# Recurrent attention and a mixture of experts in one kernel: waits moved off TensorE, another order of the opening, and split scores for the fourth unit

## The reference

```python
m_new = np.maximum(f_gate[:, :, t] + m, i_gate[:, :, t])
f_stab = np.exp(f_gate[:, :, t] + m - m_new)
i_stab = np.exp(i_gate[:, :, t] - m_new)
C = f_stab[:, :, None, None] * C + i_stab[:, :, None, None] * np.einsum('bhd,bhe->bhde', vt, kt)
n = f_stab[:, :, None] * n + i_stab[:, :, None] * kt
h_tilde = np.einsum('bhde,bhe->bhd', C, qt)
denom = np.maximum(np.abs(nq), 1.0)          # nq = n . q
y[:, :, t] = sigmoid(o_gate[:, :, t]) * h_tilde / denom
...
h = np.maximum(x @ w1[e], 0.0)               # for each of 4 experts
out += p[:, e:e + 1] * (h @ w2[e])           # p: domain_probs, normalised
```

## Time and profile before

| | |
|---|---|
| median of 3 runs | 418.74 us (417.88 to 418.81) |
| the profiled execution's own time | 418.08 us |
| its span, first to last instruction | 416.4 us |
| outside the span | 1.7 us |
| PE busy | 411.6 us, 99% |
| PE weight loads | 398.3 us, 96% |
| DVE, ACT, POOL busy | 43%, 38%, 37% |

### The profile page before, as it was taken

The page is one execution under the profiler, slowest core; times in us unless marked ns, Lnnn a source line. Parts: engine busy times, 40 slices in busy tenths (PEclk is TensorE's granted clock), DMA queues, the critical chain, the costliest instruction groups (busy, mean ns, idle before and its releaser), DMA issues.

```text
span 416.4 us, 7050 instructions
## 1 busy us (share of the span) xinstructions
PE 411.6 (99%) x2710; PEld 398.3 (96%) x2710; DVE 180.6 (43%) x372; ACT 158.5 (38%) x329; POOL 152.3 (37%) x189
## 2 busy tenths in 40 slices
PE   8999999999999999999999999999999999999997
PEld 8899999999999999999999999999999999999996
DVE  5875796646555556446223232323113132311313
ACT  4575477745355653514112431144211333211111
POOL 4865735595174925304011660065100453000000
PEclk9999999999999999999999999999999999999999
DMA  7999939678513845300000231024200000000101
GB/s 269 272 283 394 369 100 354 226 256 290 189 37 131 303 132 193 122 2 0 2 0 2 85 129 67 0 71 139 71 0 2 0 0 2 34 0 2 63 0 65
DMA packets 16899, 48.45 MB, mean 116 GB/s; under 512 B 1921, under 2 KB 8594, under 8 KB 15714
## 3 DMA queue, kind: packets, MB, share of 16 engines
q1 hardware_dynamic: 16290, 46.60, 31.9%
q10 hardware_dynamic: 576, 1.40, 1.0%
HBM read 45.94 MB, written 2.05 MB: 115 GB/s over the span
## 4 chain that ended last, share of the span: by engine, by line
PE 98%; DVE 1%; issue 0%; DVEq 0%
PE hid_ps L1076 42%; PE acc_ps L1095 37%; PE out_ps L1032 5%; PE score_ps L1095 3%; PE acc_ps L1076 2%; PE out_ps L1039 2%; PE score_ps L976 2%; PE add_ps L1011 1%; PE hid_ps L925 1%; PE score_ps L971 1%; PE acc_ps L1032 0%; PE out_ps L1051 0%; PE out_ps L1052 0%; PE out_ps L1053 0%; PE score_ps L989 0%
## 5 line engine op out<-in xcount | busy, mean ns | idle before, releaser
L810 DVE SCALAR_TENSOR_TENSOR h_lo<-hid_ps,h_hi 128x384 fp32r<-128x384 f32 (+2 forms) x120 | 68.0, 567 | 219.7 <-ACT h_hi L587 219.6
L587 ACT ACTIVATE h_hi<-hid_ps 128x384 fp32r<-128x384 f32 (+2 forms) x120 | 59.6, 497 | 231.9 <-PE hid_ps L1076 231.8
L1095 PE MATMUL acc_ps<-w_hi,h_hi 128*128 128x320 f32 x352 | 110.2, 313 | 0.0
L1095 PE MATMUL acc_ps<-w_hi,h_lo 128*128 128x320 f32 x352 | 108.8, 309 | 0.0
L1095 PE MATMUL acc_ps<-w_lo,h_hi 128*128 128x320 f32 x352 | 108.4, 308 | 0.0
L1076 PE MATMUL hid_ps<-xt_hi,w_hi 128*128 128x384 f32 (+2 forms) x360 | 104.1, 343 | 0.1
L1076 PE MATMUL hid_ps<-xt_hi,w_lo 128*128 128x384 f32 (+2 forms) x360 | 103.7, 342 | 0.0
L441 POOL TENSOR_TENSOR w_lo<-w_raw,w_hi 128x384 fp32r<-128x384 f32 x56 | 58.9, 1054 | 114.5 <-ACT w_hi L573 114.5
L1076 PEld LDWEIGHTS hid_ps<-xt_hi,w_lo 128*128 128x128 f32 x360 | 65.4, 189 | 4.3
L1095 PEld LDWEIGHTS acc_ps<-w_hi,h_hi 128*128 128x128 f32 x352 | 66.3, 188 | 1.3
L1095 PEld LDWEIGHTS acc_ps<-w_lo,h_hi 128*128 128x128 f32 x352 | 66.3, 188 | 1.3
(11 more groups left out here) (172 smaller groups left out, 371.9 us busy)
## 6 DMA issues: line engine op xcount, KB each, us to landing
w_raw<-in_w_b SPq DMA_DIRECT2D x27, 704.0 KB, 4.3
raw<-in_qk_s SPq DMA_DIRECT2D x8, 1024.0 KB
g_all<-g_dram SPq DMA_DIRECT2D x10, 512.0 KB, 6.1
kv<-in_kv_n SPq DMA_DIRECT2D x12, 352.0 KB, 5.9
q_pack<-in_q_p SPq DMA_DIRECT2D x10, 192.0 KB, 6.1
out_y<-y_acc SPq DMA_DIRECT2D x12, 160.0 KB, 1.8
carry<-g_dram SPq DMA_DIRECT2D x30, 60.0 KB
y_acc<-in_o_n SPq DMA_DIRECT2D x1, 1280.0 KB, 12.3
```

The source lines that it names most:

```text
L587: nc.scalar.activation(h_hi[:, M % RING, 0:cols], hid_bank(M)[:, 0:cols], ACT.Relu).then_inc(hid_hi, 1)
L810: nc.vector.scalar_tensor_tensor(h_lo[:, M % RING, 0:cols], hid_bank(M)[:, 0:cols], 0.0, h_hi[:, M % RING, 0:cols].bitcast(fp32), ALU.max, ...
L1095: last = nc.tensor.matmul(acc_ps[t][:, 0:DM], x, w, start=(f == 0 and i == 0), stop=(f == NF - 1 and i == 2))
```

## The change

It has four parts.

1. **Waits.** `up` no longer waits for `hid_lo` (that the hidden bank's last reader is done); an assertion in the program says that a `down` before it has waited for as much. It waits for `xt_hi_done` and `xt_done` only where a group brings new tiles. `scores` waits once per unit for its input. `additions` and `outputs` of units from 2 on wait for the keys' weights, the probabilities and the scaled queries alone; what else they waited for is now waited for by DVE ahead of the second `probs` of the unit, and by POOL ahead of `weigh_keys` and `scale_q`. Counted over the whole program, PE has 668 waits before and 432 now, and the waits beyond one at an instruction, which stand in its sequencer as instructions of their own, are 185 before and 73 now.
2. **The opening.** PE moves the chunk ends and starts (`move_ends`, `move_starts`) before the first scores, runs `keep_clock(6)` between the first scores and `outputs(0)`, and turns the first keys into another bank (`hid_ps[0]` in place of `acc_ps[2]`), copied by ACT (`first_keys`) in place of DVE. DVE does `unit_maxima` before the four first `probs`, then `unit_steps` (from POOL) and `gate_scan(1)`, then both `gate_x`. POOL does `unit_sums` between the two `weigh_keys`. ACT rounds weight blocks 2 and 3 before the first transposes, and opens output gates 2 and 3 between the two first `relu`.
3. **Unit 3.** NS is 3 in place of 4: unit 3 takes the layout `qk_s`, with CAST in slots 3 and 4 and SUB in 4 and 5. Its input is loaded on ACT's queue in the opening (`load_scores(act, 3)`, 1 MB), not on SP's after `load_g(3)` (0.4 MB in two transfers). SP issues weight pair 3 before it waits for the stored gates.
4. **Rows.** `state` and `split_qk` have 120 partitions in place of 128, and the state's product in `outputs` runs over the 120 or 80 rows that are in use. Four memsets go (two of POOL's, for unit 3's old layout; one of DVE's, for the rows left out; POOL's memset of `state` covers 120 partitions).

```diff
-NS = 4
+NS = 3
+CAST = {3: (3, 4), 4: (11, 12), ...
+SUB = {3: (4, 5), 4: (13, 14), ...
-OPEN_IN = {3: (2,), 13: (4,), 14: (6,), 17: (8,), 18: (10,)}
+OPEN_IN = {13: (4,), 14: (6,), 17: (8,), 18: (10,)}
...
             sp.dma_start(g_dram[1, NU:NU + 1, :], gate_tiles[1]["gg"][0:1, 1, :]).then_inc(gate_tiles[1]["stored"], 16)
-            load_q(3)
+            load_pair(sp, 3)
             sp.wait_ge(gate_tiles[1]["stored"], 3 * 16)
             load_g(2)
+            load_carry(2)
+            load_q(3)
             sp.wait_ge(out_done, 1)
             sp.wait_ge(add_done, 1)
             load_kv(sp, 2)
-            load_carry(2)
-            load_pair(sp, 3)
             load_g(3)
-            reload_scores(3)
...
+            def first_keys():
+                gt = gate_tiles[0]
+                act.wait_ge(gt["key_ps"], 1)
+                nc.scalar.activation(key_w[:, 0:U0], hid_ps[0][:, U0:2 * U0], ACT.Copy).then_inc(gt["key_tok"], 1)
...
             split_high(1, None)
+            first_keys()
             act.dma_start(y_acc[:, 2:4, :], o_n[:, 2:4, :]).then_inc(o_in[1], 16)
             act.dma_start(dp[:, :, :], dom_p).then_inc(dp_in, 16)
+            load_scores(act, 3)
+            split_high(2, None)
+            split_high(3, None)
             xt_high(0)
             xt_high(1)
-            split_high(2, None)
-            split_high(3, None)
             relu(0)
+            gate_open(2)
             relu(1)
...
                 wait_if(dve, out_done, k - 1)
+                if k >= B and half == 1:
+                    dve.wait_ge(fresh_ready, k)
+                    dve.wait_ge(xt_done, k)
+                if k == B and half == 1:
+                    dve.wait_ge(decay_step, 3)
...
             local_maxima()
             unit_starts()
+            unit_maxima()
...
             probs(0, 0)
             probs(0, 1)
-            unit_maxima()
             probs(1, 0)
             probs(1, 1)
-            copy_keys(0, 0, U0, acc_ps[2])
+            unit_steps()
+            gate_scan(1)
             gate_x(0)
-            gate_scan(1)
             gate_x(1)
...
                 if first_of_load(M):
                     pe.wait_ge(w_hi_done, NF * load + f + 1)
-                if f == 0:
+                if f == 0 and new_tiles(M // NF):
                     pe.wait_ge(xt_hi_done, first + tiles)
-                wait_if(pe, hid_lo, hid_free(M))
...
             exponents_first(0, 1)
+            move_ends()
             exponents_first(1, 0)
             exponents_first(1, 1)
-            move_ends()
+            move_starts()
             first_scores(0)
-            move_starts()
             first_scores(1)
+            pe.wait_ge(m_begun, 1)
+            keep_clock(6)
             outputs(0)
             pe.wait_ge(g0["exp"], 1)
             pe.wait_ge(g0["w_tok"], 1)
-            turn(g0, "key", acc_ps[2], U0, U0, "key_ps")
+            turn(g0, "key", hid_ps[0], U0, U0, "key_ps")
             outputs(1)
             transpose_x(0)
             additions(0)
+            pe.wait_ge(g0["key_tok"], 1)
             keep_clock(2)
```

More of the change, by code:

```diff
@@ L71, in begun_in, with down_before, new_tiles @@
     return None if M == EARLY - 2 or ahead >= SLOTS else ahead
+def down_before(M):
+    slots = [at for at in range(SLOTS) if begun_in(at) == M]
+    return slots[0] if slots else 0
+def new_tiles(at):
+    return at == 0 or GROUPS[at][1] + GROUPS[at][2] > max(g[1] + g[2] for g in GROUPS[:at])
 def hid_free(M):
@@ L231, in build @@
         d_exp, d_masked, p_ready = sem("d_exp"), sem("d_masked"), sem("p_ready")
-        mask_turn, ones_set, apart_set = sem("mask_turn"), sem("ones_set"), [sem(f"apart_set{i}") for i in range(2)]
+        mask_turn, ones_set, apart_set = sem("mask_turn"), sem("ones_set"), sem("apart_set")
         kv_ones, unit_step, first_in = sem("kv_ones"), sem("unit_step"), [sem(f"first_in{i}") for i in range(B)]
@@ L265, in scores_in @@
         def scores_in(k):
-            return 16 * (k // 2 + 1)
+            return 16 * sum(2 if u < NS else 1 for u in range(B + k % 2, k + 1, 2))
         def load_kv(eng, k):
@@ L366, in _ @@
                     reload_scores(5)
-                if (k := unit_at(M, -2)) is not None and NS <= k < NT - 2:
+                if (k := unit_at(M, -2)) is not None and NS < k < NT - 2:
                     reload_scores(k + 2)
@@ L563, in cast @@
                 wait_if(act, s_ready, 2 * (k - 2) + 2)
-                nc.scalar.activation(split_qk[:, kept(k), t, :, :], raw[:, kept(k), t, :, :], ACT.Copy)\
+                nc.scalar.activation(split_qk[:, kept(k), t, :, :], raw[0:KS, kept(k), t, :, :], ACT.Copy)\
                     .then_inc(cast_done, 1)
@@ L684, in copy_tokens, with later_keys @@
                 nc.vector.tensor_copy(w_tok[:, first:first + rows], bank[:, 0:rows]).then_inc(gt["w_tok"], 1)
-            def copy_keys(n, first, rows, bank):
-                gt = gate_tiles[n]
+            def later_keys():
+                gt = gate_tiles[1]
                 dve.wait_ge(gt["key_ps"], 1)
-                nc.vector.tensor_copy(key_w[:, first:first + rows], bank[:, rows:2 * rows]).then_inc(gt["key_tok"], 1)
+                nc.vector.tensor_copy(key_w[:, U0:NU], out_ps[:, U1:2 * U1]).then_inc(gt["key_tok"], 1)
             dve.wait_ge(m_first, 1)
@@ L961, in scores @@
                     pe.wait_ge(p_ready, 2 * k + half)
-                if k < NS:
+                if k < NS and half == 0:
                     pe.wait_ge(qk_in[kept(k)], scores_in(k))
-                else:
+                    pe.wait_ge(apart_set, 2)
+                elif half == 0:
                     pe.wait_ge(sub_done, 2 * (k - NS) + 2)
                 if k < NS:
-                    pe.wait_ge(apart_set[kept(k)], 2)
                     for j in range(2):
@@ L1017, in outputs @@
                 bank = out_bank.get(k, out_ps)
-                pe.wait_ge(p_ready, 2 * k + 2)
-                pe.wait_ge(kv_ones, k + 1)
-                pe.wait_ge(pool_init, 3)
+                if k < B:
+                    pe.wait_ge(p_ready, 2 * k + 2)
+                    pe.wait_ge(kv_ones, k + 1)
+                    pe.wait_ge(pool_init, 3)
                 if k == 0:
@@ L1073, in up @@
                         pe.wait_ge(w_lo_done, NF * load + f + 1)
-                    if i == 4 and f == 0:
+                    if i == 4 and f == 0 and new_tiles(M // NF):
                         pe.wait_ge(xt_done, first + tiles)
```

73 lines of the change are left out of this document (32 added, 41 removed).

## The result

The changed kernel takes 420.19 us (median of 20 runs, 418.83 to 423.48); the kernel before took 418.77 in the same call (20 runs, 416.82 to 419.99). The ratio is 1.0047, 95% interval 1.0028 to 1.0066: slower by 1.4 us, outside the predicted range of 416.9 to 419.3. The ratio is not the quotient of the two medians (1.0034), because it goes with the means, and the longer executions put these 2.0 us apart (420.64 and 418.66); three executions of 506 to 1435 us in the runs further down, one each of the kernel before, of e1 and of e4, are left out of the ratios there and move the medians by under 0.1 us. The profiled execution took 420.48 us, 2.40 more than that of before.

The account below looks back on a forecast made before the run. PE, busy 99%, was taken to bound the kernel. Opening +0.8, unit 3 −0.84 and waits −0.3 summed to −0.34 us, from a median of 418.74 to 418.4 us; 8-in-10 range 416.9 to 419.3.

Parts of the forecast that it names:

- rival C: Early transfers collide: g_all for unit 2 landing 3 us later costs PE about 2.2 us, 420.6 us; chance 8%.
- Cost on PE 0: Transfers: moving unit 3's larger input and weight pair 3 into the opening costs PE nothing.
- block 8's weights should land some us before 36.19: Transfers, with pair 3 early: ACT's 4.54 us of idle before rounding block 8 should go.
- the forecast 0.84: Unit 3's scores on PE: the split form saves 0.42 us a half, 0.84 us a unit, give or take 0.05.
- 0 to 1.3: Scores of slot 6: us that would show if unit 3's added ACT and DVE work did not fit.
- +0.8: Opening, at outputs(1) and through to the experts: 0.8 us later, from +1.15 and −0.36; bounds +0.5 and +1.1.
- Rival A: Opening gets no longer since the six products fill a hole: −1.5 us, 417.2 us; beyond −1.26 us this way, 25%.
- B: Rival on the steady part: PE's waits are in the open, removing them saves 5 to 11 us, 408 to 414; chance 3%.
- The −0.3 us for the early slots: Waits removed around up(6) and up(8): 0.3 us less; bounds −0.1 if the weights stay late, and −0.5.
- −0.34: Whole kernel: sum of opening +0.8, unit 3 −0.84 and waits −0.3, in us.
- no reserve: Slot 6: up(6) has no slack, so each us of delay in g_all is one on blocks 5 and 6.

Follow-up runs that it names:

- e1: Kernel before with only SP's new transfer order (weight pair 3 ahead of the wait for the stored gates), unit 3 whole: 418.38 us, ratio 0.9997.
- e4: Kernel before with unit 3 split, pair 3 ahead of the stored gates and unit 3's 1 MB ahead of g of unit 3: 419.06 us, ratio 1.0011.
- c1: Changed kernel with unit 3 whole as before (0.4 MB issued by SP), pair 3 still early: 418.86 us, ratio 1.0018.
- the last run above: Changed kernel with unit 3's 1 MB on SP ahead of g of unit 3, both roundings in slot 3, both subtractions in slot 4: 418.43 us, ratio 1.0014.
- b2: Kernel before with unit 3 split and nothing else, its 1 MB issued by SP at the place of the 0.4 MB: 420.07 us, ratio 1.0043.
- a2: Changed kernel without keep_clock(6) before the first sums: 419.63 us, ratio 1.0024.

## Why the prediction was wrong

The mechanism that decided was named, as rival C, and given 8%; the sum took its price as nothing.

**Transfers: the step that failed.** "Cost on PE 0", and "block 8's weights should land some us before 36.19". I read the windows as room (169 GB/s from 18 to 21 us) and did not ask what else is in that room: the stores of the gates, which SP waits for before everything that follows. They took 5.67 us in place of 2.44, `g_all` landed 2.9 us later, and PE lost 1.10 + 0.59 + 0.27 us of idle and with the slow restarts 2.54 us; C had 2.2 for 3 us. Block 8's weights landed at 35.4, 0.8 us earlier, and nothing was waiting for that. With unit 3 whole and its 1 MB away, everything else of the change costs 0.3 us by the medians (c1); with them it costs 1.4.

**Unit 3.** The gain was sized rightly: from the scores' start to the second product of the next `down` it is now

```profile
41.57 0.64 PE L998 MATMUL score_ps<-split_qk 120*128 120x128 f32 x4
42.04 0.36 PE L1114 MATMUL acc_ps<-w_hi,h_hi 128*128 128x320 f32 x1
42.23 0.31 PE L1114 MATMUL acc_ps<-w_lo,h_hi 128*128 128x320 f32 x1
```

0.66 us (0.60 in the last run above) against the 1.01 of the earlier trace rows, and 0.40 against 0.87 from the start of the second half to the transposes behind it: 0.82 us for the forecast 0.84. The price was not: "between 30 and 36 us ACT is busy 1.65 and DVE 2.24 of 6 us, so both fit" counts busy time. ACT works in order, and had spent those microseconds waiting for pair 4. The rounding behind it was free only in an order in which nothing ahead of it waits. The split alone with its bytes cost 1.5 us net (b2), so its price was 2.3 us, where I had allowed 0 to 1.3.

**Opening.** +0.8 predicted at `outputs(1)` and the first `up`, +0.72 measured against the turn. `outputs(0)` 12.43 for "near 12.9" is the turn's 0.5 us; `outputs(1)` had no idle, as said. The parts came out as forecast: `outputs(0)` 1.22 us later behind the turn (6.40 for 5.18) where I had 1.15, and `outputs(1)` 1.97 behind it in place of 2.49, a gain of 0.52 where I had 0.36. Rival A (the six products fill a hole) is out as a time. Its mechanism is half there, though: without the six products PE stands idle 0.57 us for DVE (a2), so next to that kernel they cost 0.73 us and not 1.35. That hole is one which the change itself opens.

**Waits.** 0 in the steady part, right; B is out. The −0.3 us for the early slots was tied to block 8; PE was late there for other reasons, and the run with the waits alone is too coarse to show a term of that size.

**Rows and memsets.** Not tried alone; the steps of PE's state products are unchanged.

**The sum.** −0.34 was forecast; the medians differ by 1.4 and the profiled pair by 2.4. The profiled kernel before was a quick one of its kind (418.08, median 418.77), and the gap between the two differences is likely in it: in other executions PE waits for weights with no part of the change there (excess 0.55 in the profiled one of before, 2.2 in the one with only the waits changed). I had read "no reserve" from the earlier trace rows and still taken one execution's transfers as fixed.

## What to carry to other kernels

A stretch with free DMA bandwidth is only free if nothing small and waited-for is in it: before a large transfer is moved there, look for the stores and reloads that a queue waits on, and read the time from their issue to the next issue behind them. Work given to an engine that is "busy 27%" comes no earlier than what stands ahead of it in that engine's order, so ask what each instruction ahead of it waits for. And where PE is 99% busy, an early PE does not help while the weights come at their own pace; the excess of its steps, place by place, says more than its busy share.
